# Routing of the first expert at the handover from attention: other engines, other order, single-tile places, a held-back load

## The reference

```
q, k, v: (4, 8, 576, 64)        x = attention(q, k, v), thresholded at row max - tau
x: (2304, 512)                  tokens x (heads * head_dim)
logits = x @ w_gate;  noisy = logits + log1p(exp(x @ w_noise)) * noise      (8 experts)
top2 = the two largest of noisy;  weights = softmax over the two
out1[token] = sum over its two experts e:  weight * relu(x @ w1[e]) @ w2[e]
h = out1 @ w_in;  g = max(h, 0) + alpha * min(h, 0);  result = g @ w_out
```

## Time and profile before

| | us |
|---|---|
| median of 3 runs | 1276.12 |
| the three runs | 1276.11, 1276.12, 1277.69 |
| the profiled execution | 1278.04 |
| its span on the core | 1276.3 |

### The profile page before, as it was taken

How to read it: one execution, slowest core, us unless ns; L and a number is a source line. 1 busy time by engine, 2 the same in 40 slices (tenths; PEclk the granted TensorE clock), 3 DMA queues, 4 the chain that set the end, 5 groups by cost and what they waited for, 6 DMA issues and landing times.

```text
span 1276.3 us, 20214 instructions
## 1 busy us (share of the span) xinstructions
PE 1233.1 (97%) x7666; PEld 1128.8 (88%) x7666; DVE 624.1 (49%) x1254; ACT 531.0 (42%) x953; POOL 570.7 (45%) x411
## 2 busy tenths in 40 slices
PE   7999999999989999999999999999999999999998
PEld 6899999999868889999989998988999999899997
DVE  7888888888778112121212112125454536445443
ACT  6777787777752333233323334323221112112211
POOL 7999999999650635253343434444510101000000
PEclk8999999999989899999999999999999999999999
DMA  6545454544340433342434334353321102000000
GB/s 190 136 129 141 121 149 114 142 121 130 112 113 15 150 115 132 100 149 76 156 95 135 122 101 140 100 158 116 105 65 38 34 1 75 16 0 25 17 1 25
DMA packets 71408, 123.11 MB, mean 96 GB/s; under 512 B 11936, under 2 KB 30880, under 8 KB 71328
## 3 DMA queue, kind: packets, MB, share of 16 engines
q1 hardware_dynamic: 57856, 87.69, 24.0%
q0 software_dynamic: 6080, 19.93, 4.9%
q10 hardware_dynamic: 7392, 14.42, 3.0%
HBM read 82.43 MB, written 19.92 MB: 80 GB/s over the span
## 4 chain that ended last, share of the span: by engine, by line
PE 83%; POOL 6%; ACT 5%; DVE 3%; issue 2%; DMA 1%; ACTq 0%; DVEq 0%
PE h_ps L772 32%; PE y_ps L789 11%; PE y_ps L790 10%; PE y_ps L791 10%; PE o_acc L628 6%; POOL probs_lo L1476 3%; PE ring L579 2%; PE ring L592 2%; PE ring L580 2%; PE ring L593 2%; PE t_ps L750 2%; ACT probs_hi L888 1%; ACT qk_parts L896 1%; POOL region_a L1486 1%; ACT probs L880 1%
## 5 line engine op out<-in xcount | busy, mean ns | idle before, releaser
L772 PE MATMUL h_ps<-x_hi,region_a 128*128 128x384 f32 (+1 forms) x1408 | 338.8, 313 | 3.7 <-DVE x_lo L1368 3.7
L772 PEld LDWEIGHTS h_ps<-x_hi,region_a 128*128 128x128 f32 x1408 | 244.0, 189 | 9.4 <-DVE x_lo L1368 4.3
L1476 POOL TENSOR_TENSOR probs_lo<-probs,probs_hi 128x576 fp32r<-128x576 f32 x160 | 226.7, 1426 | 41.4 <-ACT probs_hi L888 41.2
L772 PE MATMUL h_ps<-x_lo,region_a 128*128 128x384 f32 (+1 forms) x704 | 218.7, 311 | 0.0
L1378 DVE SCALAR_TENSOR_TENSOR h_lo<-h_ps,h_hi 128x256 fp32r<-128x256 f32 (+1 forms) x128 | 62.6, 490 | 302.1 <-ACT h_hi L993 302.1
L996 ACT ACTIVATE h_hi<-act_out 128x384 fp32r<-128x384 f32 (+1 forms) x112 | 53.7, 480 | 305.9 <-DVE act_out L1389 305.9
L789 PE MATMUL y_ps<-region_b,h_hi 128*128 128x512 f32 x436 | 172.5, 396 | 1.5 <-DVE h_lo L1395 1.5
L791 PE MATMUL y_ps<-region_b,h_lo 128*128 128x512 f32 x436 | 170.8, 392 | 0.0
L790 PE MATMUL y_ps<-region_b,h_hi 128*128 128x512 f32 x436 | 170.8, 392 | 0.0
L1462 POOL TENSOR_TENSOR region_b<-stage,region_b 128x1024 fp32r<-128x1024 f32 x40 | 95.8, 2398 | 141.2 <-ACT region_b L869 141.1
L993 ACT ACTIVATE h_hi<-h_ps 128x256 fp32r<-128x256 f32 (+1 forms) x128 | 55.8, 437 | 237.7 <-PE h_ps L772 233.4
(11 more groups left out here) (241 smaller groups left out, 2408.2 us busy)
## 6 DMA issues: line engine op xcount, KB each, us to landing
stage<-in_moe_w SPq DMA_DIRECT2D x56, 512.0 KB, 3.7
qk_parts<-qk_parts SPq DMA_DIRECT2D x120, 160.0 KB, 2.5
qk_raw<-in_qk SPq DMA_DIRECT2D x32, 320.0 KB, 3.4
expert_rows<-rows_out ACTq DMA_DIRECT2D x8, 768.0 KB, 3.8
v_nat<-in_v SPq DMA_DIRECT2D x16, 320.0 KB, 3.3
early<-in_moe_w SPq DMA_DIRECT2D x16, 256.0 KB, 4.3
x_rows<-stage SPq DMA_DIRECT2D x16, 256.0 KB, 3.0
expert_rows<-rows_out ACTq DMA_DIRECT2D x8, 512.0 KB, 2.8
```

The costliest lines, as they stand in the source:

```text
L772: mm = pe.matmul(h_ps[:, c % 2, 0:width], wt, x[kind][:, cc, :], start=(n == 0), stop=(n == 3 * C - 1))
L1476: pool.tensor_tensor(probs_lo[:, m % 4, :], probs[:, m % 4, :], probs_hi[:, m % 4, :].bitcast(F32), ALU.subtract).then_inc(lo_done, 1)
```

## The change

Five edits, all at the handover and in the routing:

1. The three noisy-logit operations of the 12 early tiles go from VectorE (slot 161) to POOL (slot 158, behind the probs_lo of tile 157). For this ACT makes a Relu as well, since POOL adds and multiplies only.
2. TensorE's counts and marks stand ahead of the products with V of tile 159, in the same slot. Its sums L700 stand ahead of the first two turned groups.
3. VectorE makes the places in slot 162, ahead of den, rden and x_head. They are one tensor_scalar for each tile (12, and 36 in `place_rows`), with the tile's value as a pointer scalar, and partition_at is now bf16. The semaphores count tiles.
4. One linked step less: the counts are added into an int32 tile directly.
5. SP waits for the third gather of expert 0 before alpha and the weights of expert 1.

```diff
@@ SP
             sp.dma_start(x_early[:, FIRST_TILES:TOK, DM - 2 * D:DM], late_rows[:, :, DM - 2 * D:DM]).then_inc(x_in[1], 16)
+            sp.wait_ge(ex["gathered"][UT[0] - 1], 16)
             sp.dma_start(alpha_sb[:, :], alpha.rearrange("(f p) -> p f", p=P), allow_slow_non_contiguous=True).then_inc(alpha_in, 16)
@@ PE, slot: the block "if tile(i, c) == FIRST_COUNTS_AT" now stands ahead of "if has(i, c - LAG, TILES, SL)"
@@ PE, handover
-            pe.wait_ge(x_in[0], 16)
-            turn_late(0)
-            turn_late(1)
             pe.wait_ge(first_tokens_ready, 2)
...
-                    pe.wait_ge(first_at_ready, 1 if q == 0 else 2)
+                    pe.wait_ge(first_at_ready, FIRST_TILES // 2 if q == 0 else FIRST_TILES)
...
             mm.then_inc(first_summed, 1)
+            pe.wait_ge(x_in[0], 16)
+            turn_late(0)
+            turn_late(1)
@@ ACT
                     soft_terms(0, first_terms["neg"], first_terms["exp"], first_terms["log"])
+                    act.activation(first_terms["soft"], first_terms["logits"][:, :, E:2 * E], ACT.Relu).then_inc(first_relu, 1)
@@ DVE
-                noisy_logits(F_["logits"], F_["log"], noise_sb[:, 0:FIRST_TILES, :], F_["soft"], F_["tmp"], F_["noisy"])
+                dve.wait_ge(first_noisy, 3)
...
-                link(dve.tensor_tensor(all_(F_["f"]), first_ps[:, 0:FIRST_TILES], all_(F_["far"]), ALU.add))
-                link(dve.tensor_copy(all_(F_["i"]), all_(F_["f"])))
+                link(dve.tensor_tensor(all_(F_["i"]), first_ps[:, 0:FIRST_TILES], all_(F_["far"]), ALU.add))
...
-                for a, b in ((0, FIRST_TILES // 2), (FIRST_TILES // 2, FIRST_TILES)):
-                    dve.tensor_tensor(at_partition_first[:, a:b, :], over_tiles(partition_at[:, :], b - a), wide(F_["p"][:, a:b], P),
-                                      ALU.is_equal).then_inc(first_at_ready, 1)
+                for t in range(FIRST_TILES):
+                    dve.tensor_scalar(at_partition_first[:, t, :], partition_at, F_["p"][:, t:t + 1], None, ALU.is_equal).then_inc(first_at_ready, 1)
...
-                dve.tensor_tensor(at_partition[:, q:q + TOK // 2, :], over_tiles(partition_at[:, :], TOK // 2),
-                                  wide(slot_p[:, q:q + TOK // 2], P), ALU.is_equal).then_inc(at_partition_ready, 1)
+                for t in range(q, q + TOK // 2):
+                    dve.tensor_scalar(at_partition[:, t, :], partition_at, slot_p[:, t:t + 1], None, ALU.is_equal).then_inc(at_partition_ready, 1)
@@ POOL, slot 158
+                pool.wait_ge(route_act, 2)
+                pool.wait_ge(first_relu, 1)
+                pool.wait_ge(route_in, 48)
+                pool.tensor_tensor(F_["tmp"], F_["soft"], F_["log"], ALU.add).then_inc(first_noisy, 1)
+                pool.wait_ge(first_noisy, 1)
+                pool.tensor_tensor(F_["log"], F_["tmp"], noise_sb[:, 0:FIRST_TILES, :], ALU.mult).then_inc(first_noisy, 1)
+                pool.wait_ge(first_noisy, 2)
+                pool.tensor_tensor(F_["noisy"], F_["log"], F_["logits"][:, :, 0:E], ALU.add).then_inc(first_noisy, 1)
```

More of the change, by code:

```diff
@@ L218, in build @@
         w_parts_hi = sem("w_parts_hi"); w_parts_lo = sem("w_parts_lo");
-        first_mask_ready = sem("first_mask_ready"); first_counted = sem("first_counted"); first_marks = sem("first_marks"); first_tokens_ready = sem("first_tokens_ready"); first_at_ready = sem("first_at_ready")
+        first_mask_ready = sem("first_mask_ready"); first_relu = sem("first_relu"); first_noisy = sem("first_noisy"); first_counted = sem("first_counted"); first_marks = sem("first_marks"); first_tokens_ready = sem("first_tokens_ready"); first_at_ready = sem("first_at_ready")
         first_summed = sem("first_summed"); first_idx_ready = sem("first_idx_ready")
@@ L613, in slot @@
                     mm.then_inc(pair_turned, 1)
+                if tile(i, c) == FIRST_COUNTS_AT:
+                    pe.wait_ge(freed, last_use - 1)
+                    pe.wait_ge(route_pool, 2)
+                    pe.wait_ge(first_mask_ready, 1)
+                    pe.matmul(first_ps[:, 0:FIRST_TILES], lower[:, :], first_mask[:, :], start=True, stop=False)
+                    for d in range(1, FIRST_TILES):
+                        mm = pe.matmul(first_ps[:, d:FIRST_TILES], ones_bf[:, :], first_mask[:, 0:FIRST_TILES - d],
+                                       start=False, stop=(d == FIRST_TILES - 1))
+                    mm.then_inc(first_counted, 1)
+                    pe.wait_ge(first_marks, 1)
+                    pe.matmul(marks_ps[:, 0:1], ones_bf[:, :], marks_bf[:, :], start=True, stop=True).then_inc(first_counted, 1)
                 if has(i, c - LAG, TILES, SL):
@@ L636, in slot @@
                     mm.then_inc(first_logits_ready, 1)
[L637 to L647, removed]
                 f = max_rows_in(i, c)
@@ L1115, in first_expert_slots @@
                 dve.wait_ge(first_counted, 1)
[L1116 to L1117 removed]
+                link(dve.tensor_tensor(all_(F_["i"]), first_ps[:, 0:FIRST_TILES], all_(F_["far"]), ALU.add))
                 link(dve.tensor_scalar(all_(F_["p_i"]), all_(F_["i"]), P - 1, None, ALU.bitwise_and))
+                link(dve.tensor_tensor(all_(F_["c"]), all_(F_["i"]), all_(F_["p_i"]), ALU.subtract))
                 link(dve.tensor_copy(all_(F_["p"]), all_(F_["p_i"])))
[L1120 removed]
                 link(dve.tensor_tensor(column_first[:, :, :], over_tiles(column_at[:, 0:UT[0]], FIRST_TILES), wide(F_["c"], UT[0]), ALU.is_equal))
@@ L1219, in slot_and_routing @@
                     first_expert_slots()
-                if tile(i, c) == FIRST_COUNTS_AT + 1:
                     first_expert_places()
@@ L1488, in _, with first_noisy_logits @@
             float_iota = lambda out, pattern, **k: pool.iota(out, pattern, allow_small_or_imprecise_dtypes=True, **k).then_inc(route_pool, 1)
+            def first_noisy_logits():
+                F_ = first_terms
+                pool.wait_ge(route_act, 2)
[6 more added lines that the diff above has]
+                pool.tensor_tensor(F_["noisy"], F_["log"], F_["logits"][:, :, 0:E], ALU.add).then_inc(first_noisy, 1)
             def slot_and_weights(i, c):
                 slot(i, c)
+                if tile(i, c) == FIRST_LOGITS_AT + 1:
+                    first_noisy_logits()
                 if tile(i, c) == PAIR_AT + 8:
```

11 lines of the change are left out of this document (4 added, 7 removed).

## The result

| | us |
|---|---|
| the kernel before, median of 18 runs | 1276.99 (1274.11 to 1278.80) |
| the changed kernel, median of 18 runs | 1279.44 (1277.53 to 1280.81) |
| ratio, 95% interval | 1.0021 (1.0015 to 1.0027): +2.7 us, 1.9 to 3.5 |
| its profiled execution, span | 1279.38, 1277.5 |
| the changed kernel again, 12 runs on another occasion (e11) | ratio 1.0013 (0.9999 to 1.0026): +1.7 us |

The changed kernel is about 2 us slower. Single traces are shifted against each other from the start, so I count from one event that the change doesn't touch: the start of the last full exponential of tile 158 on ACT. These are the two rows, before (L880) and after (L881); the columns of a timeline are start, us, operation, idle before.

What follows compares the result with a forecast made beforehand. TensorE was taken as busy 97% of the span, with the chain over VectorE at the handover from attention to experts. Mask 0, alpha +0.5 and places +0.9 summed to +1.4 us: 1277.5 us, range 1274.5 to 1280.6.

Steps and rivals of the forecast that it cites:

- Noisy logits, mask: Early tiles' noisy logits on POOL: VectorE's mask still waits for POOL's moved-back work; 0 us taken, between 0 and -0.9.
- Counts ahead of the last products: TensorE's counts delay the last head's copy and transposes, hidden before VectorE's den: no cost; up to 1.2 us without that cover.
- Twelve places: First expert's places on VectorE as twelve tensor_scalars: 0.165 us from start to start, 2.1 us together.
- x_head (+1.95) and idx_first (-0.4): On VectorE, x_head behind the places ends at 374.5, before 372.54; idx_first comes at 374.85 for 375.24.
- Late block: TensorE resumes its work on the last six tiles of x between -0.1 and +0.3 us; -0.1 taken.
- Landing of the late rows: Load of x's last rows, issued at 377.5, lands 3.9 us later at 381.4, just hidden before TensorE needs it.
- Alpha: Alpha, held behind the third gather, lands at 385.4 after 3.65 us, delaying VectorE's x_lo and the first expert: +0.5 us.
- Places of all tiles: Routing: 36 VectorE operations for four make TensorE wait about 1.05 us in the sums for 0.17: +0.9 us.
- Rival 3: Third gather lands after 5.4 us, alpha after 5.2, first expert begins at 390.4: 1280.5 us, chance 0.14.
- Rivals 1 and 2: First: cheap VectorE steps, 1274.6 us, chance 0.12; second: the same plus TensorE sooner at full clock, 1273.2, chance 0.11.
- Rival 4: TensorE's wait in the sums of the places grows to 1 to 3 us and its clock falls: 1280.5, chance 0.10.
- Rival 5: Nothing moves, since VectorE's wait on POOL is the same before and after: 1276.1 us, chance 0.06.

Runs made afterwards that it cites:

- e11: The changed kernel again, unchanged, 12 runs on another occasion: ratio 1.0013 (0.9999 to 1.0026) to the kernel before, +1.7 us.
- e10: Changed kernel with VectorE's wait for alpha moved to the last layer, weights still held: ratio 1.0013 (1.0002 to 1.0024) to the kernel before.
- e4: Changed kernel with x_head made ahead of the first expert's places, which stay tile by tile: ratio 1.0019 (1.0010 to 1.0028) to the kernel before.
- e3: Changed kernel with the places of all tiles again as four operations over nine tiles each: ratio 1.0009 (1.0000 to 1.0017) to the kernel before.
- e1: Changed kernel without SyncE's wait for the third gather before alpha and expert 1's weights: ratio 1.0018 (1.0008 to 1.0029) to the kernel before.
- e8: Kernel before with only the changed orders (counts, sums and places moved ahead), nothing held back: ratio 1.0008 (0.9997 to 1.0019).
- e5: Kernel before with only the early tiles' noisy logits on POOL, with ACT's Relu: ratio 1.0002 (0.9990 to 1.0013).
- e6: Kernel before with only alpha and expert 1's weights held behind the third gather: ratio 1.0011 (0.9998 to 1.0024).
- e7: Kernel before with only the places made tile by tile, partition_at in bf16: ratio 1.0003 (0.9992 to 1.0015).
- e9: Kernel before with four late groups turned before the sums, first h_lo earlier, alpha's wait at the last layer, alpha and expert 1's weights held: ratio 0.9978 (0.9966 to 0.9990).
- e12: The e9 kernel without its hold, so alpha and expert 1's weights follow right behind the late rows: ratio 1.0003 (0.9993 to 1.0012) to the kernel before.
- e2: Changed kernel with alpha issued ahead of SyncE's wait, only expert 1's weights held: ratio 1.0015 (1.0005 to 1.0025) to the kernel before.

## Why the prediction was right, and where it wasn't

The forecast was +1.4 us, 1277.5; measured were 1279.44, inside the range, with +2.7 (1.9 to 3.5), and +1.7 in e11. That is a small loss at the very border of 0.2%. Of the 1.94 us between the forecast and the measured median, 0.87 is the kernel before itself, whose median was 1276.12 in three runs and 1276.99 in 18. The sign and the two large terms hold, both sizes were off by some tenths, and the mechanism of one was only half of it: alpha, which carries the +0.5 of the sum, is worth at most 0.05 us when it is taken out (e10). That the number is as near as this is partly luck, for the path that was put at nothing ends at the same moment as the one that was priced.

- **Noisy logits, mask (0, bounds 0 to -0.9).** -0.2. The choice between held and not held was the right one: L1096, with one SBUF input, ends 0.03 us behind POOL's second probs_lo. POOL's price was right too: 0.40, 0.39 and 0.39 us; the gaps between them were 0.07 us, and the three took 1.33 us for 1.4.
- **Counts ahead of the last products (0, hidden).** Hidden for den, as I said, since den then waits for the places. It isn't free, though: in e4, where x_head is first, it delays x_head by 0.42 us.
- **Twelve places (2.1 us, 0.165 each).** 2.04, 0.163 from start to start. The nearest row, L1122, was the right one to go by.
- **x_head (+1.95) and idx_first (-0.4).** +1.75 and -0.7.
- **Late block (-0.1).** It ran dry at +18.35 for +19.10, so 0.75 sooner. 0.36 is from the earlier restart, the rest from the clock, which rose 1.6 us sooner in this trace and gave the block's end back at 2.4 GHz; in e11 it is +17.9.
- **Landing of the late rows.** Here the step failed: "lands 3.9 later at 381.4 ... so this is just hidden". 3.9 us was read from a row where the load went out ahead of the gathers. Now the gathers start at 374.02, 375.46 and 376.71, around the load's 376.44, and it takes 4.8 to 5.3 us with the hold (changed, e3, e10, e11) and 5.4 to 5.7 without (e1, e8). Where it goes out ahead of them it takes 3.4 to 3.9 (before, e5, e6, e7, e9, e12). That the gathers are what slows it is argued from this order; no run has this load without them. With 3.9 it would have landed 0.4 us after TensorE had run dry, with 5.1 TensorE waited 1.66 us. "Each further delay would count in full" was right.
- **Alpha (+0.5).** It landed in 3.0 us, sooner than the 3.65 I took, and the third gather in 5.5, later than 3.9. VectorE waited as foreseen, and this chain alone would have given some +1.0. But the late rows' is as long: e10 takes alpha's away and gains at most 0.05 us, e4 takes the late rows' away and gains 0.6 until alpha stops it. Neither alone is the cause; in e8, with alpha not held back, the late rows alone make +1.44.
- **Places of all tiles (+0.9).** 0.73: TensorE waits 0.91 us for 0.17. The wait was expected at 1.05.
- **Sum.** 1.03 + 0.73 = 1.76 us for 1.4; the rest of the measured +2.7 may lie in how many executions have a lower mean clock, which isn't shown. Whoever had gone by the forecast's cause and taken the hold away would have got the first expert another 0.4 to 0.5 us later.

Rival 3 had the gather's landing right (5.5 us for its 5.4), but not alpha's. Rivals 1 and 2 needed steps of 0.07 to 0.1 us, and an operation of this form costs 0.163; the sooner clock of rival 2 is there in part, but behind it TensorE only waits longer for the late rows. Rival 4 doesn't come true in this trace: TensorE waits 0.91 us before the last nine sums, and its granted clock is 1.00 in 410 to 412 us. Rival 5 has the mask right and the orders wrong. The Trainium skill, VectorE: DVE Perf Modes, The TRN2 errata, gives 58 + 128/4 cycles, an estimate of 0.094 us; below its table it says that a measured fixed part was nearer 150 cycles, and with that the estimate is 0.19 us. A single operation here is 0.249 us, and 0.163 from start to start. For L1096 the rows show 0.98 us beside POOL, and 0.17 in e9, where POOL is idle:

```profile
368.00 0.17 DVE L1098 TENSOR_SCALAR first_mask<-qk_raw 128x12 bf16<-128x12 f32 x1
```

The Trainium skill, SBUF — State Buffer, SBUF: two separate sides, says that of a GpSimd operation and a VectorE operation in a 2-port perf mode, or with two SBUF inputs, the one that starts first keeps the shared ports for its whole instruction. The trace agrees, as L1096 ends with POOL's instruction; in which mode it ran the profile doesn't show.

## What to carry to other kernels

Before an operation is moved ahead of another, list what the second one sets free on other queues: here 1.75 us of delay for x_head bought 0.7 us for the indices, and x_head had a store, a load and TensorE behind it. Take a DMA's landing time from a row with the same neighbours, and ask of each transfer what will now be in flight with it. Relieve the engine that sets the end first: holding loads back gave nothing in the kernel before, where TensorE was late, and about 1.9 us, without the clock's part, after a needless wait of TensorE was gone. And take two traces of one kernel before a stretch at the lower clock is put down to an edit.

## What the runs showed of the hardware

- A load of 8 KB right behind another one may delay it as much as 8 KB and 1 MB of weights together do. In e2, one trace, alpha (2048 values, each 4 bytes by itself) alone followed the late rows, and they landed in 5.7 us, as in e1 with the weights; with alpha held they took 4.8 to 5.3. Alpha itself took 6.5 us there, and 2.7 to 3.0 behind the hold.
- A VectorE operation of 12 columns with one SBUF input was held to the end of POOL's instruction, 0.98 us for 0.17.
- A second stretch at 1.2 GHz, 3.4 us long (6.8 in e12), stands at the first expert or just ahead of it in seven of fourteen traces. Two traces of the same code differ in it, and it goes neither with TensorE's waits for a DMA (none behind 2.26 us in e1, one in e5 behind 0.28 us) nor with the change.
